# Expert routing tile by tile into lists of token numbers, with blocks gathered by number

## The chip, the cores and the metric

The kernel runs on one core of a Trainium2 chip. It is fp32 throughout: where the matmul wants precision, a number is split into a rounded part ("hi") and a remainder ("lo"), and three products (hi·hi, hi·lo, lo·hi) are added. The metric is the device time of one execution in microseconds (us). The kernel before takes 1038.77 us, the median of 3 runs (1036.66 to 1042.51).

## The reference

Three layers follow each other. Tokens are numbered b·768 + t for 4 batches of 768.

```python
# 1. linear attention with a delta rule, per batch and head (4 x 8 heads of 48), 768 steps
y[t] = q[t] @ state;  v_old = kt @ state;  state += bt * outer(kt, v[t] - v_old)
# 2. dense layer on 3072 tokens of 384
h = x @ w_in; x = np.maximum(0.01 * h, h) @ w_out          # 384 -> 2048 -> 384
# 3. one expert of 8 for each token
logits = x @ w_gate + modality_bias[modality_id]
e_idx = np.argmax(logits, axis=1); gate_w = softmax(logits)[n, e_idx]
for e in range(8):
    mask = e_idx == e
    out[mask] = gate_w[mask, None] * (np.maximum(x[mask] @ w1[e], 0) @ w2[e])   # 384 -> 1024 -> 384
```

The reference's own numbers for these inputs put 3069 tokens on expert 1 and 3 on expert 3; the other six get none. In blocks of 128 tokens that is 24 + 1 = 25 blocks.

## The kernel before

Every engine has an instruction stream written out by hand, with semaphores between them. Two nested loops, `for n, f in slots(): slot(n, f)`, order the first two layers. n is a tile of 512 tokens (6 tiles, `TT`; 128 tokens of each batch), f one of 16 slices of the 2048 hidden features. In slot (n, f) TensorE (PE) runs `up(n, f + 1)` (9 matmuls of 512 columns), pieces of the attention of tile n + 1 and n + 2, and `down(n, f)` (9 matmuls). So attention is spread between the matmuls of the dense layer. The last tile, n = 5, has no attention beside it. After each `up`, ACT scales (`small_h`), DVE takes the maximum (`leaky`), ACT rounds (`round_g`) and DVE makes the remainder (`rest_g`); `down` needs that.

The small steps on PE share three PSUM banks (5, 6, 7) in rotation. `fill(step)` takes the next bank and waits until the step that used it three turns earlier has been drained (`drained0` to `drained2`); the engine that reads the bank signals that. In slot 8 these steps are two W, one Y and two K transposes (KT), in slot 9 two U (`updates`) and two KT.

Routing: `rows_t` and `logits_half` transpose the result of tile n - 1 and compute its logits in slots 0 to 4 of tile n. All other routing waits for the last tile. Then DVE chooses experts for all 24 groups of 128 tokens at once, PE computes ranks, DVE forms each token's row in the sorted order (`pos`), and GpSimd (POOL) writes 24 groups of rows to `sorted_rows` in DRAM, one indirect DMA for each:

```python
for j in range(TOKT):
    pool.indirect_dma_start(out=sorted_rows, out_offset=...(ap=pos[:, j:j + 1], axis=0), in_=row_buf[:, j, :]).then_inc(s.scat, 16)
```

Meanwhile DVE makes the block table (a column per block: expert, count, change, next expert, active, end) and signals `tab_rdy`. SP loads the first expert's weights, waits for all 24 scatters and loads block 0 and block 1.

The expert stage is a loop over blocks of 128 sorted rows. `pe_block(x)` runs `block_up(x)` (18 matmuls), the transposes of the next block `block_t(x + 1)`, `block_down(x - 1)` (24 matmuls) and `block_ht(x)` (8 transposes). DVE and ACT split the results; DVE copies the row's token number and gate to `meta` and signals `meta_rdy`. That lets SP load block x + 2 with one plain DMA, since sorted rows are contiguous. POOL scatters finished rows to `out`. When the expert changes, ACT and DVE split new weights, and POOL takes half of the w2 split.

Of the kernel before, what the change touches and what calls it, by code (L numbers as in the profile page):

```python
# [14 lines left out]
P = 128  # L15
# [26 lines left out]
ROW = DM + 4  # L42
MODS = 2

# [47 lines left out]
def build(nc, q, k, v, beta, moe_w_in, moe_w_out, modality_id, w_gate, modality_bias, w1, w2, out):  # L92
    with ExitStack() as ctx:
# [6 lines left out]
        x2_rows = nc.dram_tensor("x2_rows", [TOKT, P, DM], F32, kind="Internal").ap()  # L100
        wo_lo_d = nc.dram_tensor("wo_lo_d", [FT, P, DM], F32, kind="Internal").ap()
        sorted_rows = nc.dram_tensor("sorted_rows", [(BLOCKS + 2) * P, ROW], F32, kind="Internal").ap()
# [7 lines left out]
        empty_row = sb("empty_row", [P, ROW])  # L110
# [3 lines left out]
        lx = sb("lx", [P, TOKT, EXPERTS])  # L114
        mask = sb("mask", [P, CH])
        after_constants = sb.at
# [11 lines left out]
        x2_t = sb("x2_t", [P, KT, TW])  # L128
        g_hi = [sb(f"g_hi{i}", [P, TW], F32R) for i in range(2)]
        g_raw, g_lo = [], []  # L130
        for i in range(2):
# [25 lines left out]
        mask2 = nc.alloc_sbuf_tensor_at("mask2", [P, P], F32, offset=SB_END - 4 * P)  # L157
        assert sb.at <= SB_END - 4 * P


        sb = Region(nc, attention_at)
        row_buf = sb("row_buf", [P, TOKT, ROW])
        before = sb("before", [P, P])
        ones = sb("ones", [P, P])
        lg, bsel, eq, onehot, within = (sb(x, [P, TOKT, EXPERTS]) for x in ("lg", "bsel", "eq", "onehot", "within"))

        PAD_T, PAD_E = 16, 4
        pref = [sb(f"pref{i}", [P, PAD_T + TOKT, EXPERTS]) for i in range(2)]
        end_sum = [sb(f"end_sum{i}", [P, PAD_E + EXPERTS]) for i in range(2)]
        modf, mod0, mx, total, gate, emin, posf = (sb(x, [P, TOKT]) for x in  # L170
                                                   ("modf", "mod0", "mx", "total", "gate", "emin", "posf"))
        pos = sb("pos", [P, TOKT], I32)
        iota_e = sb("iota_e", [P, EXPERTS])
        iota_i = sb("iota_i", [P, EXPERTS], I32)
        token_id = sb("token_id", [P, TOKT], I32)
        blk_i = sb("blk_i", [P, EXPERTS], I32)
        blk_j = sb("blk_j", [P, EXPERTS], I32)
        blk_n, start, used, last_e = (sb(x, [P, EXPERTS]) for x in ("blk_n", "start", "used", "last_e"))
        NBK = BLOCKS + 1
        bi_i = sb("bi_i", [1, NBK], I32)  # L180
        bi_f = sb("bi_f", [1, NBK])
        be_tmp = sb("be_tmp", [1, NBK, EXPERTS])
        be_tmp2 = sb("be_tmp2", [1, NBK, EXPERTS])
# [1346 lines left out]
```

## Time and profile before

| | |
|---|---|
| median of 3 runs | 1038.77 us |
| profiled execution | 1043.0 us, span 1041.2 us |
| busy share: PE / DVE / ACT / POOL | 87% / 52% / 33% / 6% |
| dense layer ends, first expert matmul | 717.98 us, 773.88 us |
| chain of waits, by engine | PE 73%, DVE 15%, ACT 3% |

All times below are of the profiled execution, from the start of its span. The busy share says who works most over the whole span; which stage a change can shorten is read from the chain of waits and from stretches of time.

### The profile page before, as it was taken

What the parts mean: (1) busy time and instruction counts of PE and PEld (TensorE: products, weight loads), DVE (VectorE), ACT (ScalarE), POOL (GpSimd) and SP (SyncE); (2) the same over time, 40 slices, a digit from 0 to 9 for tenths busy, and PEclk for the clock granted to TensorE, in tenths of its full rate; (3) what the DMA queues carried; (4) which work ended last, traced back from release to release, by engine and by line L of the source; (5) the groups of instructions that cost most, each with busy time, mean ns of one, the idle gap of its engine ahead of it and who ended that gap; (6) DMA issues with size and microseconds to landing.
All of it is one profiled execution on the core that took longest, in us unless ns stands there. A gap on an engine that the chain in (4) does not pass through costs nothing.

```text
span 1041.2 us, 26308 instructions
## 1 busy us (share of the span) xinstructions
PE 910.7 (87%) x10264; PEld 781.9 (75%) x10265; DVE 542.5 (52%) x1455; ACT 344.8 (33%) x608; POOL 66.7 (6%) x79
## 2 busy tenths in 40 slices
PE   5195899989999999999999999998039999999982
PEld 5194678878887888888888887886028999999972
DVE  5947963688249843885378523243523333333341
ACT  4153244433344344424443423333022222222240
POOL 0000000000000000000000000000550101110111
PEclk9677989999999999999999999999559999999995
DMA  9311544454024402351225012250471111111122
GB/s 202 99 35 39 130 126 149 148 151 111 25 55 107 115 26 62 92 123 33 55 63 127 28 32 69 69 197 16 162 265 54 46 38 38 46 38 46 38 91 76
DMA packets 151745, 89.04 MB, mean 86 GB/s; under 512 B 108385, under 2 KB 147809, under 8 KB 151265
## 3 DMA queue, kind: packets, MB, share of 16 engines
q1 hardware_dynamic: 148512, 78.14, 28.0%
q0 software_dynamic: 3136, 9.49, 2.3%
q8 instruction: 75, 1.23, 0.5%
q14 instruction: 22, 0.17, 0.1%
HBM read 59.77 MB, written 23.32 MB: 80 GB/s over the span
## 4 chain that ended last, share of the span: by engine, by line
PE 73%; DVE 15%; ACT 3%; issue 2%; POOL 2%; SPq 1%; DMA 1%; POOLq 0%; DVEq 0%; ACTq 0%
PE bank L462 16%; PE bank L447 15%; PE bank L638 10%; PE bank L614 10%; DVE inv_t L1193 3%; DVE inv_tmp L1187 3%; PE bank L406 2%; PE bank L391 2%; POOL sorted_rows L866 2%; PE bank L624 2%; PE bank L338 2%; PE bank L433 2%; PE bank L430 2%; PE bank L477 2%; PE bank L418 2%
## 5 line engine op out<-in xcount | busy, mean ns | idle before, releaser
L1255 DVE TENSOR_TENSOR g_raw<-bank,g_raw 128x512 f32<-128x512 f32 x96 | 66.2, 689 | 151.7 <-ACT g_raw L963 151.4
L963 ACT ACTIVATE g_raw<-bank 128x512 f32<-128x512 f32 x96 | 57.3, 597 | 250.2 <-PE bank L447 250.2
L462 PE MATMUL bank<-g_hi,wo_hi 128*128 128x512 f32 x288 | 121.9, 423 | 9.5 <-DVE g_lo L1259 7.5
L447 PE MATMUL bank<-x_hi,wi_hi 128*128 128x512 f32 x288 | 117.2, 407 | 12.5 <-DVE x_lo L1251 12.5
L462 PE MATMUL bank<-g_lo,wo_hi 128*128 128x512 f32 x288 | 113.9, 395 | 0.0
L462 PE MATMUL bank<-g_hi,wo_lo 128*128 128x512 f32 x288 | 113.6, 395 | 0.0
L447 PE MATMUL bank<-x_lo,wi_hi 128*128 128x512 f32 x288 | 113.4, 394 | 0.0
L447 PE MATMUL bank<-x_hi,wi_lo 128*128 128x512 f32 x288 | 113.3, 393 | 0.0
L968 ACT ACTIVATE g_hi<-g_raw 128x512 fp32r<-128x512 f32 x96 | 60.6, 631 | 89.7 <-DVE g_raw L1255 89.7
L1259 DVE TENSOR_TENSOR g_lo<-g_raw,g_hi 128x512 fp32r<-128x512 f32 x96 | 66.2, 690 | 41.7 <-ACT g_hi L968 41.6
L638 PE MATMUL bank<-w_hi,ht_hi 128*128 128x384 f32 x200 | 70.4, 352 | 7.6 <-DVE ht_lo L1481 7.2
L1193 DVE TENSOR_TENSOR inv_t<-inv_t,inv_tmp 128x110 f32<-128x110 f32 (+35 forms) x366 | 75.3, 247 | 0.2
L1187 DVE TENSOR_TENSOR inv_tmp<-inv_a,inv_t 128x110 f32<-128x110 f32 (+35 forms) x366 | 74.9, 246 | 0.0
L447 PEld LDWEIGHTS bank<-x_hi,wi_hi 128*128 128x128 f32 x288 | 54.7, 190 | 25.4 <-DVE x_lo L1251 13.4
L462 PEld LDWEIGHTS bank<-g_hi,wo_hi 128*128 128x128 f32 x288 | 54.5, 189 | 23.3 <-issue 9.1
L638 PE MATMUL bank<-w_lo,ht_hi 128*128 128x384 f32 x200 | 68.2, 341 | 0.0
L638 PE MATMUL bank<-w_hi,ht_lo 128*128 128x384 f32 x200 | 68.0, 340 | 0.0
L462 PEld LDWEIGHTS bank<-g_lo,wo_hi 128*128 128x128 f32 x288 | 54.6, 190 | 12.4
L447 PEld LDWEIGHTS bank<-x_hi,wi_lo 128*128 128x128 f32 x288 | 54.7, 190 | 11.9
L614 PE MATMUL bank<-w_hi,xt_hi 128*128 128x512 f32 x150 | 61.7, 412 | 1.6 <-DVE xt_lo L1452 1.2
L447 PEld LDWEIGHTS bank<-x_lo,wi_hi 128*128 128x128 f32 x288 | 54.9, 190 | 10.4
L462 PEld LDWEIGHTS bank<-g_hi,wo_lo 128*128 128x128 f32 x288 | 54.8, 190 | 8.8
(199 smaller groups left out, 1568.5 us busy)
## 6 DMA issues: line engine op xcount, KB each, us to landing
wo_lo<-wo_lo_d SPq DMA_DIRECT2D x80, 192.0 KB, 2.4
w_raw<-in_moe_w SPq DMA_DIRECT2D x6, 1536.0 KB, 7.9
sorted_rows<-empty_row SPq DMA_DIRECT2D x33, 194.0 KB, 2.9
xb<-sorted_rows SPq DMA_DIRECT2D x27, 194.0 KB, 2.4
kq_in_rows<-in_k SPq DMA_DIRECT2D x6, 768.0 KB, 5.2
k_raw<-in_k SPq DMA_DIRECT2D x24, 192.0 KB, 4.1
vals<-in_v SPq DMA_DIRECT2D x24, 192.0 KB, 4.4
kq_in_rows<-in_q SPq DMA_DIRECT2D x6, 768.0 KB, 5.3
```

Source lines behind the costliest of these rows:

```text
L338: mm = pe.matmul(b[half_p(hh), CH * j:CH * j + CH], k_t[head_p(hh), pair, chunk(m // 2)], k_t[head_p(hh), pair, chunk(m // 2)], start=True ...
L391: mm = pe.matmul(b[half_p(hh), HD * j:HD * j + HD], k_t[head_p(hh), pair, chunk(c)], state[c][head_p(hh), pair, :], start=True, stop=True)
L447: mm = pe.matmul(bank[f % 2][:], a[:, m, P * f:P * f + P], x[:, m, :], start=(m == 0 and x is x_hi and a is wi_hi), stop=(m == KT - 1 and ...
L462: mm = pe.matmul(acc[m][:], w[:, P * m:P * m + P], g[f % 2][:], start=(f == 0 and g is g_hi and w is not wo_lo[j % RING]), stop=(f == FT - ...
L614: mm = pe.matmul(bank[2 + h][:], a[par][:, m, :], w[:, m, 512 * h:512 * h + 512], start=(m == 0 and a is xt_hi and w is w1_hi), stop=(m == ...
L638: mm = pe.matmul(bank[6 + par][:, 0:DM], a[:, m, :], w[:, m, :], start=(m == 0 and a is ht_hi and w is w2_hi), stop=(m == KE - 1 and a is ...
L963: act.activation(g_raw[f % 2][:], bank[f % 2][:], ACT.Copy, scale=0.01).then_inc(s.hs_ev, 1)
L968: act.activation(g_hi[f % 2][:], g_raw[f % 2][:], ACT.Copy).then_inc(s.gh_ev, 1)
L1187: made.append(counted(dve.tensor_tensor(tmp[:, a:b, :], inv_a[:, j, j + 1 + a:j + 1 + b].unsqueeze(2).broadcast_to([P, b - a, cols]), inv_ ...
L1193: c = counted(dve.tensor_tensor(rows_t, rows_t, tmp[:, a:b, :], ALU.add))
L1255: dve.tensor_tensor(g_raw[f % 2][:], bank[f % 2][:], g_raw[f % 2][:], ALU.max).then_inc(s.gr_ev, 1)
L1259: dve.tensor_tensor(g_lo[f % 2][:], g_raw[f % 2][:], g_hi[f % 2][:].bitcast(F32), ALU.subtract).then_inc(s.g_rdy, 1)
```

## The change

The choice of expert, ranks and places are done for each tile in the slots of the next tile. Expert e owns a fixed range of a list in DRAM, `id_list`, from e · 4096. `place` turns ranks into list positions with a running `base`, and POOL scatters pairs of token numbers (8 bytes) to these positions, four indirect DMAs a tile. The rows themselves stay in `x2_rows` in DRAM in tile order, now 385 wide with the gate in the last column. A block is read in two steps: SP loads 128 pairs of numbers (`load_ids`), and POOL gathers the 128 rows by number. After five tiles `first_expert` takes the expert with most tokens so far; its weights are loaded and split in the slots of the last tile, and its first two blocks are run without the table. `block_table` follows behind them. POOL's half of the w2 split goes to DVE. The writes of empty rows (33 DMAs) and the reload of `row_buf` are gone.

```diff
+        id_list = nc.dram_tensor("id_list", [LIST, 2], I32, kind="Internal").ap()
@@ tensor
+            def ranks(n):
+                pe.wait_ge(s.picked_rdy, n + 1)
+                b, done = fill(("K", n))
+                pe.matmul(b[:, 0:SUB * EXPERTS], lower[:], picked[:, SUB - 1:, :].rearrange("p a b -> p (a b)"), start=True, stop=False)
+                for d in range(1, SUB):
+                    pe.matmul(b[:, 0:SUB * EXPERTS], ones[:], picked[:, SUB - 1 - d:2 * SUB - 1 - d, :].rearrange("p a b -> p (a b)"),
+                              start=False, stop=(d == SUB - 1))
+                for i in range(SUB):
+                    mm = pe.matmul(b[:, 64:64 + EXPERTS], ones[:], picked[:, SUB - 1 + i, :], start=(i == 0), stop=(i == SUB - 1))
+                mm.then_inc(done, 1)
...
+                late = 0 if n == TT - 1 else 3
+                if n >= 1 and f in (late, late + 1):
+                    logits(n - 1, f - late)
+                if n >= 1 and f == (3 if n == TT - 1 else 8):
+                    ranks(n - 1)
...
+                if n == TT - 1 and f == FT - 2:
+                    pe.wait_ge(s.gr_ev, FT * TT - 1)
+                    block_t(Blk(0, 0))
...
+            logits(TT - 1, 0)
+            logits(TT - 1, 1)
             for i in range(SUB):
                 rows_t(TT - 1, i)
+            ranks(TT - 1)
+            block_up(Blk(0, 0), 1)
+            pe.wait_ge(s.gr_ev, FT * TT)
+            block_t(Blk(0, 1))
...
+            block_ht(0)
+            block_up(Blk(0, 1), 1)
+            block_down(Blk(0, 0), 1)
+            block_ht(1)
+            block_t(Blk(0, 2))
             pe.wait_ge(s.tab_rdy, 1)
+            block_up(Blk(0, 2))
+            block_t(Blk(0, 3))
+            block_down(Blk(0, 1))
+            block_ht(2)
@@ sync
+            def load_ids(x, at):
+                sp.dma_start(ids[x.par][:], id_list[bass.ds(at, P), :]).then_inc(ids_in[x.par], 16)
...
+                if n >= 1 and f == (6 if n == TT - 1 else 11):
+                    store_gates(n - 1)
+                if n == TT - 1 and f == 5:
+                    sp.wait_ge(s.first_rdy, 1)
+                    first = sp.value_load(first_i[0:1, 0:1], min_val=0, max_val=EXPERTS - 1)
+                    load_w1(first)
+                    load_w2(first)
+                if n == TT - 1 and f == 7:
+                    sp.wait_ge(s.scat, 16 * SUB * (TT - 1))
+                    for x in (Blk(0, 0), Blk(0, 1)):
+                        load_ids(x, sp.value_load(first_i[0:1, 1 + x.n:2 + x.n], min_val=0, max_val=LIST - P))
...
-                sp.wait_ge(s.meta_rdy, b + 1)
-                load_block(x.next(2))
+                sp.wait_ge(s.meta_rdy, x.n + 1)
+                load_ids(x.next(2), list_at(sp, x.next(2)))
...
+            load_ids(Blk(0, 2), list_at(sp, Blk(0, 2)))
+            load_next(1, sp.value_load(table[0:1, 3, 0:1], min_val=0, max_val=EXPERTS - 1))
@@ gpsimd
+            def gather(x, rows=TOKENS):
+                pool.wait_ge(ids_in[x.par], x.half * 16 + 16)
+                pool.sem_inc(s.gather_go, 1)
+                pool.indirect_dma_start(out=xb[x.par][:], out_offset=None, in_=x2_rows[0:rows, :], in_offset=bass.IndirectOffsetOnAxis(
+                    ap=ids[x.par][:, 0:1], axis=0), bounds_check=last_token, oob_is_err=False).then_inc(xb_in[x.par], 16)
...
-                        pool_block(Blk(i, d))
+                        gather(Blk(i, d).next(2))
                         scatter(Blk(i, d - 1))
@@ vector
+            def place(n):
...
+                step(dve.tensor_tensor(at_e[:], b[:, 0:SUB * EXPERTS].rearrange("p (a b) -> p a b", b=EXPERTS), over_j(base[:], SUB),
+                                       ALU.add))
+                dve.tensor_tensor(base[:], base[:], b[:, 64:64 + EXPERTS], ALU.add).then_inc(drain(("K", n)), 1)
+                step(dve.tensor_tensor(at_e[:], at_e[:], picked[:, SUB - 1:, :].bitcast(F32), ALU.mult))
+                step(dve.tensor_reduce(posf[:], at_e[:], AX.X, ALU.add))
+                dve.tensor_copy(pos[:, tile], posf[:]).then_inc(s.pos_rdy, 1)
...
+                if n >= 1 and f == (4 if n == TT - 1 else 9):
+                    place(n - 1)
+                if n == TT - 1 and f == 4:
+                    first_expert()
+                if n == TT - 1 and f in (9, 10):
+                    split_w1(f - 9, 1)
+                if n == TT - 1 and f in (11, 12):
+                    split_w2(f - 11, 1)
...
+            relu(0)
+            split_xt(Blk(0, 1))
+            keep_meta(Blk(0, 0))
+            split_ht(0)
+            block_table()
+            relu(1)
+            keep_meta(Blk(0, 1))
+            gated(Blk(0, 0))
+            split_ht(1)
+            split_xt(Blk(0, 2))
```

Three places show how instructions move. The first is PE in slots 8 and 9 of tile 1. Of the kernel before, this is the end of `up(1, 10)`, the two U steps of slot 9, which wait for banks of the rotation (`drained`), and the start of `down(1, 9)`:

```order
L447 MATMUL bank<-x_hi,wi_lo 128x512
L406 MATMUL bank<-vals,inv_s 64x48 [waits drained0,drained2,drained1,td_ev]
L406 MATMUL bank<-vals,inv_s 64x48 x15
L406 MATMUL bank<-vals,inv_s 64x48 [waits drained1,drained0,td_ev]
L406 MATMUL bank<-vals,inv_s 64x48 x15
L462 MATMUL bank<-g_hi_69,wo_hi 128x512 [waits g_rdy,ring1]
```

Of the change, first the end of slot 8's Y step, the ranks (L506 to L511) and the start of `down(1, 8)`, then the same place in slot 9 as above:

```order
L446 MATMUL bank<-qk_t,u_sb 48x64 x2
L506 MATMUL bank<-picked,lower 128x32 [waits drained2,picked_rdy]
L508 MATMUL bank<-picked,ones 128x32 x3
L511 MATMUL bank<-picked,ones 128x8 x4
L475 MATMUL bank<-g_hi_91,wo_hi 128x512 [waits g_rdy,ring0]
```

```order
L460 MATMUL bank<-x_hi,wi_lo 128x512
L419 MATMUL bank<-vals,inv_s 64x48 [waits drained2,drained0,td_ev]
L419 MATMUL bank<-vals,inv_s 64x48 x15
L419 MATMUL bank<-vals,inv_s 64x48 [waits drained0,td_ev]
L419 MATMUL bank<-vals,inv_s 64x48 x15
```

The ranks take one more turn of the rotation, on the bank of `drained2`; two KT steps later the first U step of slot 9 comes to the same bank, and its wait on `drained2` is for the ranks to be drained. In the kernel before, that turn of the bank belonged to the Y step of slot 8, which ACT drains.

The second is DVE in slots 9 and 10 of the same tile. Before, `leaky` (L1255) and `rest_g` (L1259) of slot 9 are followed at once by those of slot 10:

```order
L1255 TENSOR_TENSOR g_raw_71<-bank,g_raw_71 128x512 [waits hs_ev]
L1259 TENSOR_TENSOR g_lo_70<-g_raw_71,g_hi_68 128x512 [waits gh_ev]
L1255 TENSOR_TENSOR g_raw_73<-bank,g_raw_73 128x512 [waits hs_ev]
L1259 TENSOR_TENSOR g_lo_72<-g_raw_73,g_hi_69 128x512 [waits gh_ev]
L1133 COPY diag<-bank 32x256 [waits filled2]
```

Of the change (L1320 is `leaky`, L1324 `rest_g`, L1374 to L1383 `place`):

```order
L1320 TENSOR_TENSOR g_raw_94<-bank,g_raw_94 128x512 [waits hs_ev]
L1324 TENSOR_TENSOR g_lo_93<-g_raw_94,g_hi_91 128x512 [waits gh_ev]
L1374 TENSOR_TENSOR at_e<-bank,base 128x32 [waits picked_rdy,filled2]
L1376 TENSOR_TENSOR base<-base,bank 128x8 [waits route]
L1377 TENSOR_TENSOR at_e<-at_e,picked 128x32
L1378 TENSOR_REDUCE posf<-at_e 128x4 [waits route]
L1379 CAST pos<-posf 128x4 [waits route]
L1381 TENSOR_REDUCE total<-ex 128x4 [waits ex_rdy]
L1382 TENSOR_SCALAR total<-total 128x4 [waits route]
L1383 RECIPROCAL gate<-total 128x4 [waits route]
L1320 TENSOR_TENSOR g_raw_96<-bank,g_raw_96 128x512 [waits hs_ev]
```

The bank of the ranks is drained by L1376, which stands behind `rest_g` of slot 9.

The third is SP in the block loop, between the signal `meta_rdy` and the load that follows it. Before, the row address is known and the block itself is loaded (L788):

```order
L793 UNCONDITIONAL_BRANCH
L802 REGISTER_ALU
L788 ISA [waits meta_rdy]
L788 DMA xb_164<-sorted_rows 128x388
L810 UNCONDITIONAL_BRANCH
```

Of the change:

```order
L840 REGISTER_ALU
L312 ISA [waits meta_rdy]
L312 TENSOR_LOAD table
L312 ISA x2
L757 ISA
L757 DMA ids_140<-id_list 128x2
```

Behind the wait stand a value load and its two checks, and what is loaded is the block's numbers; the block's rows follow by POOL's gather.

## Rows read from the trace of the kernel before

**Rows 1.** The page: busy us (share of the span) and instructions of each engine.
```profile
PE 910.7 (87%) x10264; PEld 781.9 (75%) x10265; DVE 542.5 (52%) x1455; ACT 344.8 (33%) x608; POOL 66.7 (6%) x79
```
**Rows 2.** Stretches: length, busy PE, PEld, DVE, ACT, POOL, granted clock, DMA share, GB/s.
```profile
150.00:640.00 490.00, 484.86 (x6794) 405.04 (x6787) 291.23 (x825) 192.13 (x351) 2.86 (x3) 1.00 0.33 84
718.00:774.00 56.00, 7.74 (x44) 6.85 (x44) 22.73 (x74) 11.13 (x14) 28.62 (x25) 0.59 0.43 151
```
**Rows 3.** Chain of waits, dense layer to experts: start, us, what.
```profile
715.69 2.30 PE bank L462 x9
...
719.73 4.09 PE bank L477 x24
...
769.22 2.49 DMA xb<-sorted_rows
...
773.88 6.87 PE bank L614 x18
```
**Rows 4.** Chain of waits, one block of the expert stage.
```profile
792.22 4.12 PE bank L614 x18
796.33 0.33 PE bank L601 x3
796.66 4.17 PE bank L638 x24
800.83 0.87 PE bank L624 x8
```
**Rows 5.** Slot 9 of tile 1: chain of waits, then DVE's timeline.
```profile
284.06 2.00 PE bank L406 x64
...
286.12 0.69 DVE L1259 TENSOR_TENSOR g_lo<-g_raw,g_hi 128x512 fp32r<-128x512 f32 x1 [0.69 <-ACT g_hi L968]
```
**Rows 6.** Small operations, DVE's timeline: the table runs from 734.58 on.
```profile
723.85 0.19 DVE L1353 COPY lx<-bank 128x32 f32<-128x32 f32 x1 [8.31 <-PE bank L477]
...
734.58 0.17 DVE L1411 TENSOR_SCALAR used<-blk_n 128x8 f32<-128x8 f32 x1
...
744.06 0.17 DVE L1441 CAST table<-at_end 1x32 int32<-1x32 f32 x1
```
**Rows 7.** One block on DVE, SP and POOL, timeline.
```profile
789.08 0.17 DVE L1474 COPY meta<-xb 128x2 f32<-128x2 f32 x1 [0.58 <-issue]
789.45 0.34 SPq L788 DMA_DIRECT2D xb<-sorted_rows  x1
791.38 0.62 DVE L1461 TENSOR_SCALAR o_sb<-bank,meta 128x384 f32<-128x384 f32 x1 [2.13 <-PE bank L638]
...
792.85 1.01 POOL L876 DMA_INDIRECT out<-o_sb,meta  x1 [22.22 <-DVE o_sb L1461]
```
**Rows 8.** DMA issues over the span: count, KB each, us to landing.
```profile
xb<-sorted_rows SPq DMA_DIRECT2D x27, 194.0 KB, 2.4
...
x_rows<-stage SPq DMA_DIRECT2D x20, 192.0 KB, 1.8
...
out<-o_sb,meta POOLq DMA_INDIRECT x25, 2.5
```
**Rows 9.** Line L266, a value load from the table, 770 to 960 us, ns.
```profile
L266 SPq TENSOR_LOAD <-table x19: 263/270/275, 783.5 to 951.7; - x19
```
**Rows 10.** A large load in the last tile, and the ring load behind it.
```profile
row_buf<-x_rows SPq DMA_DIRECT2D x1, 3840.0 KB, 13.0
...
DMA to landing us min/median/max: 9.8/9.8/9.8
```
**Rows 11.** Indirect DMAs beside two weight loads, 740 to 750 us.
```profile
sorted_rows<-row_buf,pos POOLq DMA_INDIRECT x8, 4.9
```
**Rows 12.** Chain of waits: twelve logit matmuls at full clock.
```profile
665.15 1.31 PE bank L477 x12
```
**Rows 13.** DVE's timeline: two halves of w1, later one of w2.
```profile
999.33 3.43 DVE L1488 TENSOR_TENSOR w_lo<-w_raw,w_hi 128x1536 fp32r<-128x1536 f32 x2 [1.78 <-ACT w_hi L1091]
...
1014.20 3.72 DVE L1493 TENSOR_TENSOR w_lo<-w_raw,w_hi 128x1536 fp32r<-128x1536 f32 x1 [2.17 <-ACT w_hi L1079]
```

More of the change, by code:

```diff
@@ new lines, in block_t, with block_up @@
+            def block_t(x):
+                b, par = x.n, x.par
+                pe.wait_ge(xb_in[par], x.half * 16 + 16)
+                if not early(b):
+                    pe.wait_ge(s.xt_rdy, b - 1)
+                for m in range(KT):
+                    mm = pe.transpose(bank[par][:, P * m:P * m + P], xb[par][:, P * m:P * m + P], ident[:])
+                mm.then_inc(s.xt_mm, 1)
+            def block_up(x, count=None):
+                b, par = x.n, x.par
+                count = expert_count(pe, x) if count is None else count
+                pe.wait_ge(s.xt_rdy, b + 1)
+                pe.wait_ge(s.relu_a, b)
+                pe.wait_ge(s.relu_d, b)
+                for h in range(2):
+                    pe.wait_ge(w1l[h], count)
+                    for m in range(KT):
+                        for a, w in ((xt_hi, w1_hi), (xt_hi, w1_lo), (xt_lo, w1_hi)):
+                            mm = pe.matmul(bank[2 + h][:], a[par][:, m, :], w[:, m, 512 * h:512 * h + 512],
+                                           start=(m == 0 and a is xt_hi and w is w1_hi), stop=(m == KT - 1 and a is xt_lo))
+                    mm.then_inc(s.m1_mm, 1)
@@ L489, in slot, with pe_block @@
+            def pe_block(x):
+                block_up(x)
+                block_t(x.next())
+                block_down(x.next(-1))
+                block_ht(x.n)
             def slot(n, f):
@@ L642, in pe_block @@
-            def pe_block(x, first=False):
-                b, par = x.n, x.par
-                block_up(x)
-                block_t(x.next())
-                if not first:
-                    block_down(x.next(-1))
-                block_ht(b)
+            ranks(TT - 1)
+            block_up(Blk(0, 0), 1)
+            pe.wait_ge(s.gr_ev, FT * TT)
+            block_t(Blk(0, 1))
+            for i in range(SUB):
+                pe.wait_ge(*is_drained(("R", TT - 1, i)))
+            pe.wait_ge(*is_drained(("K", TT - 1)))
@@ L1455, in gated @@
+            choose(TT - 1)
+            place(TT - 1)
             def gated(x):
@@ L1460, in gated, with relu @@
                 dve.wait_ge(s.meta_rdy, b + 1)
[L1461 to L1464 removed]
+                dve.tensor_scalar(o_sb[par][:], bank[6 + par][:, 0:DM], meta[par][:, 0:1], None, ALU.mult).then_inc(s.o_rdy, 1)
+            def relu(b):
                 dve.wait_ge(s.m1_mm, b * 2 + 2)
```

728 lines of the change are left out of this document (373 added, 355 removed).

## The prediction

> **What bounds the kernel now.** I read the page first: PE is busy 87% of the span [rows 1]. Which stages the rest lies in comes from the stretches of time. From 150 to 640 us PE is busy 484.86 of 490 us, and from 718 to 774 us only 7.74 of 56 [rows 2]. So the reader should see a program that is limited by PE, with one hole of 56 us. The chain of waits shows what the hole is made of: the dense layer's last matmuls end at 717.98 us (715.69 + 2.30 in the chain, rounded), logits follow, DVE routes all tokens, POOL sends 24 scatters, block 0 is loaded at 769.22, and the first expert matmul starts at 773.88 [rows 3]. After that one block costs 4.12 + 0.33 + 4.17 + 0.87 = 9.49 us, all of it PE [rows 4], 24 times. Work that is put into the first stretch or into the block loop costs what it adds to PE's own chain. Work taken out of the hole pays in full. I sum against the profiled execution's own time of 1043.0 us. It is 4.2 us above the median of the three runs, so at the end I scale by 1038.77/1043.0.
>
> **What the first five tiles pay.** Logits are 24 matmuls a tile as before. New are 8 rank matmuls a tile, of 32 or 8 columns. The trace has no such thing. From above they cost what logit matmuls of 96 columns cost, 1.31/12 = 0.11 us each [rows 12], and from below nothing. I take 0.07, as they are narrower but load the same weights: 0.6 us a tile, 3 us in five tiles (0 to 4.4).
>
> The bank rotation costs more. In tiles 1 to 3 the first U step of slot 9 needs the ranks' bank, and that is drained by the second instruction of `place`, behind `rest_g` of that slot. U started at 284.06, right after `up`; `rest_g` ended at 286.12 + 0.69 = 286.81 [rows 5]. Two small operations behind it (0.19 us for one of 128x32 [rows 6], the second half overlapped) put the drain at 287.1. PE then stands 3.0 us with `down` queued behind U, as it issues in order. Three tiles give 9.1 us. In tile 4 there are no KT steps, so the ranks' bank comes up again only in slot 10, and in tile 5 there is no attention: nothing. The other new work hides. DVE's choice and placing (some 15 operations of 0.2 us a tile [rows 6]) lie in slots 6 and 9, beside PE's attention steps. The scatters of numbers run on an idle POOL. ACT's table changes between exponential and square root come ahead of waits. If that cover were gone, each tile would pay 1 to 3 us. The 33 writes of empty rows freed nothing that PE waited for.
>
> **The last tile.** `place` and `first_expert` are together about 16 dependent steps of 0.2 us [rows 6], 3.3 us. DVE's idle time in a slot and the slack of the `down` chain are together about as long: 0.1 us. SP waits for `first_rdy` before it issues the weights, and the next ring load of `wo_lo` (needed by `down(5, 8)`) is queued behind 3 MB of them. The row to compare is the reload of 3.84 MB in this same tile: it took 13.0 us, and a ring load issued 3.7 us later took 9.8 us, so it landed with it [rows 10]. For 3.07 MB that is 10.7 us from about 679.5, so 690.2, and by my count `down(5, 8)` would start near 689.2: 1 us of stall (0 to 3). Splitting the weights fits into ACT's and DVE's idle time there. So the dense layer ends 3 + 9.1 + 0.1 + 1 = 13.2 us later.
>
> **The hole.** Counted from the end of the dense layer (0). Logits and rows as now until 7.6: copy out 1.75, 24 logit matmuls 4.09 [rows 3], transposes. `choose` (6 steps of 0.2) ends at 7.1, so ranks run at 7.7 and `block_up(0)` starts at 9.0. It is 4.12 us at full clock [rows 4] and ends at 13.1. Relu, split, `keep_meta` and the two halves of `ht_lo` keep DVE until 16.6. Then comes `block_table`, 45 instructions. The present table has 38 in 744.23 - 734.58 = 9.65 us [rows 6], and the new one has more that overlap; I take 10.3 (9 to 11.5), until 26.9. PE meanwhile runs `up(1)` and `down(0)` until 23.2, (13.1, then 0.7 for relu, 0.9 for `block_ht`, 4.1 and 4.2), then waits for relu(1), which stands behind the table on DVE, until 27.6. SP goes on at 27.0: a value load with its checks 0.5 (0.27 is the load [rows 9]), number load 2.2, POOL's start 0.85, gather 4.9, because the next expert's weights are issued right behind (scatters beside such loads took 4.9 [rows 11]). Block 2 is there at 35.5, is transposed and split in 1.5, and `up(2)` starts at 37.0. In the kernel before, `up(2)` starts at 792.22 [rows 4], which is 74.2. That is 37.2 us gained. One part comes back: after a wait of 8 us in the sum the granted clock will be low again, as it was for the present first block, where `up` took 6.87 us [rows 3] and not 4.12: 2.7 us. Net gain 34.5.
>
> **The block loop.** Here a short plain load becomes a chain. Before, `meta` ends at 789.25, the block load is issued at 789.45 and takes 2.4 us, and the transposes need it at 796.33 [rows 4, 7, 8]. So from `meta` to the transposes there are 7.1 us. Now: 0.2 to wake SP, 0.5 for the value load [rows 9], number load 2.2, POOL from signal to issue 0.85 (o_sb ends at 792.00, POOL starts at 792.85 [rows 7]), gather, 0.1 to wake PE. The gather is not in the trace. The indirect scatter to `out` lands in 2.5 us; a plain load takes 0.6 longer than a plain store, 2.4 against 1.8 [rows 8]. So 3.1, with 2.5 and 4.9 as ends. The sum is 6.95 (6.35 to 8.75), and `meta` itself is 0.1 later for one more copy. It just fits, and since `meta(b)` also waits for the transposes of b + 1, each us above 7.1 would be paid by every block. I take 0.05 us a block, 1 us for 21 blocks.
>
> The Trainium skill (DMA: Bandwidth & Descriptors, Anatomy of one DMA, SWDGE path) gives 2.0 us plus bytes/436e3 for a DMA issued by GpSimd, 2.45 us for these 197 KB, and says the wait is longest where the target is HBM. By it the gather would be shorter than the scatter and the loop 0.65 us from its limit. The rows have it the other way for plain transfers, load slower than store, and the sum goes by them.
>
> **The end.** w2 is split by DVE alone: two halves of some 1.7, as w1's, one behind the other, instead of one of 3.72 beside POOL's work [rows 13]. With ACT's halves overlapped `down` starts 1.4 us sooner; but POOL's last gather waits for numbers queued behind a useless weight load and delays the last scatters. Together 0.
>
> **Sum.** 13.2 - 34.5 + 1 = -20.3: 1043.0 becomes 1022.7, and 1018.5 on the scale of the median. I say 1019.
>
> **Rivals.**
> - *The gather does not fit* (chance 0.22). 0.4 to 1.1 us more a block, 8 to 23 us: 1027 to 1042, the middle 1034. For it: there is no margin, and small number loads of 8 bytes a partition are unmeasured. Against: most of my pieces are from quiet rows of the same loop.
> - *The bank wait is shorter or absent* (0.10). Then 6 to 9 us less, 1010 to 1013. For it: U runs one turn after ranks only if the rotation is as I counted. Against: the order shows the same `drained2`.
> - *Slower* (0.08). One mechanism: the gather's landing at the loaded value of 4.9 us in every block. The chain is 8.75 + 0.1, 1.75 us over, times 21 is 37 us: 1055. It decides from about 0.97 us a block, a gather landing of 4.0 us. For it: rows are read in scattered order, beside a scatter. Against: in the quiet loop the scatter's landing is 2.5.
> - The forecast, 1012 to 1026 (0.60).
>
> **How the numbers follow.** About 0.5% is what a measurement of this kernel can tell from no change, 5.2 us. Faster takes the forecast, the bank rival and half and more of the first: 0.60 + 0.10 + 0.13 = 0.83. Same 0.08, slower 0.09. The range goes from 1009, where the bank rival begins, to 1035, the middle of the gather rival: it leaves out about 0.19.
>
> **What would show it.** In the profile after: PE waits of about 3 us at the U step (L419), three times, released by DVE `base`; ranks of 0.5 us or so; the first expert matmul about 9 us after the dense layer; a wait for relu of block 1 of some 4 us and one for the gather of block 2 of some 5; then a block period of 9.5 us. A wait of PE for the DMA of `xb` in each block would mean the gather rival. The prediction would be wrong above all through the landing time of the gather, which counts 21 times, and next through the table's length, which counts once.

## The result, and the profile after

The kernel before takes 1037.80 us (median of 4, 1036.66 to 1042.51), the changed one 1052.86 us (median of 4, 1051.73 to 1055.83). The ratio is 1.0141, 95% interval 1.0101 to 1.0180: slower by 1.4%, where faster by 2% was forecast. The span of the profiled execution goes from 1041.2 to 1052.0 us, 10.8 longer, where the medians are 15.1 apart: the execution profiled before was one of the longer ones of its kernel (1043.0 us against the median of 1037.80), the one profiled after was not (1053.73 against 1052.86). Stretches of the two traces therefore add up to 10.8, and some 4 us of the medians' difference is not in them.

The page of the changed kernel, busy time and granted clock:

```profile
PE 932.5 (89%) x10308; PEld 796.5 (76%) x10309; DVE 551.9 (52%) x1561; ACT 353.1 (34%) x609; POOL 85.8 (8%) x100
...
PEclk9676999999999998999899999998978999999986
```

PE is busy 21.8 us longer than before [rows 1] with 44 instructions more. Longer at nearly the same count points to slower matmuls, so the clock row is the next thing to read, and the waits of PE go with it:

```profile
PE bank L520 <- DMA xb<-x_rows,ids: 9.6, 2, 7.2
PE bank L419 <- DVE base L1376: 9.6, 3, 3.2
...
PE bank L475 <- DMA wo_lo<-wo_lo_d: 6.3, 1, 6.3
PE bank L557 <- DVE ht_lo L1593: 5.8, 1, 5.8
...
PE bank L543 <- issue: 4.0, 1, 4.0
```

The last two are no new losses: both lie in places that the forecast had. The first belongs to the change of expert near the end, where the same wait was 7.2 us before; the second ends at 778.50 us and is the wait behind the block table.

Stretches of the changed kernel, columns as in [rows 2]; the first and the last are whole stages, the three between lie behind a wait of PE:

```profile
150.00:640.00 490.00, 475.82 (x6563) 397.82 (x6555) 294.68 (x878) 196.78 (x345) 18.59 (x19) 0.98 0.34 69
...
289.90:293.30 3.40, 3.40 (x36) 2.92 (x33) 0.00 (x0) 0.95 (x2) 2.65 (x3) 0.50 0.02 1
402.60:409.40 6.80, 6.15 (x70) 5.60 (x71) 1.36 (x9) 0.49 (x1) 4.58 (x5) 0.50 0.01 1
...
716.60:723.40 6.80, 4.32 (x10) 3.45 (x11) 0.00 (x0) 0.00 (x0) 2.05 (x2) 0.50 0.45 130
751.00:790.00 39.00, 24.34 (x128) 20.94 (x128) 17.43 (x73) 8.07 (x16) 5.00 (x5) 0.80 0.31 106
```

Before, the granted clock was 1.00 from 150 to 640 us [rows 2]. Now there are stretches at 0.50, the lower level of 1.2 GHz, of 3.4 us (tile 1) and 6.8 us (tiles 2 and 3), each right behind a wait of 3.2 us, and 6.8 us around the wait for `wo_lo`. Two more, of 3.4 us each, begin at 218.2 us, at the start of tile 1, and at 641.5 us, at the end of tile 4; the kernel before has neither.

I divided both traces at the same events (the start of DVE's `x_lo` of each tile, of the first copy of `x_t` at the end of the dense layer, and of the first matmul of `up` of blocks 2 and 24; before, that of block 2 starts at 791.97 us, 0.25 ahead of its row in the chain [rows 4]). The differences add up to the span's. An ordinary table, in us:

```
                                          before    after   difference  forecast
start to x_lo of tile 1                   215.82   216.26      +0.4        0
tile 1                                    108.91   114.73      +5.8        3.6
tile 2                                    108.88   115.76      +6.9        3.6
tile 3                                    108.90   115.90      +7.0        3.6
tile 4                                    101.97   105.96      +4.0        0.6
tile 5, to the end of the dense layer      73.53    82.64      +9.1        1.7
end of the dense layer to up(2)            73.97    38.42     -35.5      -37.2
up(2) to up(24)                           209.70   215.63      +5.9        3.7
up(24) to the end                          39.52    46.73      +7.2        0
sum                                                           +10.8      -20.3
```

Nearly all of the forecast gain of the hole is there. It was lost again in five other places: slot 9 of tiles 1 to 3, tile 4, the ring load of tile 5, the block loop and the end.

Slot 9 of tile 1, the chain of waits:

```profile
279.46 0.21 PE bank L506
279.67 0.34 PE bank L508 x3
280.01 0.44 PE bank L511 x4
...
283.49 2.07 PE bank L460 x9
285.58 0.61 ACT g_raw L1003
286.21 0.70 DVE g_raw L1320
286.94 0.64 ACT g_hi L1010
287.63 0.57 issue
288.21 0.19 DVE at_e L1374
288.42 0.17 DVE base L1376
288.60 0.14 issue
288.73 2.70 PE bank L419 x64
```

The reader should see: `up` ends at 285.58, U waits until `base` frees the bank and starts at 288.73, and its 64 matmuls then take 2.70 us. At the full clock they took 2.00 [rows 5]. The ranks take 1.0 us (first three rows).

### The profile page after: what moved, and what is told of

It is laid out like the page before. It is cut to its first block, busy times and chain, and to the rows that moved or that the text cites. A ratio compares the mean times of both kernels' runs of the same rounds, so it can differ in the third digit from the quotient of the medians.

```text
span 1052.0 us, 26474 instructions
## 1 busy us (share of the span) xinstructions
PE 932.5 (89%) x10308; PEld 796.5 (76%) x10309; DVE 551.9 (52%) x1561; ACT 353.1 (34%) x609; POOL 85.8 (8%) x100
## 4 chain that ended last, share of the span: by engine, by line
PE 72%; DVE 15%; DMA 4%; ACT 3%; issue 2%; SPq 1%; DVEq 0%; POOLq 0%; POOL 0%; ACTq 0%
PE bank L475 16%; PE bank L460 15%; PE bank L533 9%; PE bank L557 9%; DVE inv_t L1258 3%; DVE inv_tmp L1252 3%; PE bank L419 3%; PE bank L404 2%; PE bank L446 2%; PE bank L443 2%; PE bank L351 2%; PE bank L543 2%; PE bank L497 2%; PE bank L431 2%; DMA wo_lo<-wo_lo_d 1%
## 5 line engine op out<-in xcount | busy, mean ns | idle before, releaser
L1320 DVE TENSOR_TENSOR g_raw<-bank,g_raw 128x512 f32<-128x512 f32 x96 | 66.0, 688 | 161.4 <-ACT g_raw L1003 158.3
L475 PE MATMUL bank<-g_hi,wo_hi 128*128 128x512 f32 x288 | 124.2, 431 | 13.3 <-DMA wo_lo<-wo_lo_d 6.3
L460 PE MATMUL bank<-x_hi,wi_hi 128*128 128x512 f32 x288 | 118.1, 410 | 10.3 <-DVE x_lo L1316 10.3
L1324 DVE TENSOR_TENSOR g_lo<-g_raw,g_hi 128x512 fp32r<-128x512 f32 x96 | 66.2, 689 | 41.7 <-ACT g_hi L1010 40.8
L460 PEld LDWEIGHTS bank<-x_hi,wi_hi 128*128 128x128 f32 x288 | 55.3, 192 | 23.5 <-DVE x_lo L1316 11.4
L882 POOL DMA_INDIRECT id_list<-row_token,pos x24 | 23.7, 986 | 542.9 <-DVE pos L1379 537.4
L460 PEld LDWEIGHTS bank<-x_lo,wi_hi 128*128 128x128 f32 x288 | 55.5, 193 | 10.7
```

Source lines behind the costliest of these rows:

```text
L460: mm = pe.matmul(bank[f % 2][:], a[:, m, P * f:P * f + P], x[:, m, :], start=(m == 0 and x is x_hi and a is wi_hi), stop=(m == KT - 1 and ...
L475: mm = pe.matmul(acc[m][:], w[:, P * m:P * m + P], g[f % 2][:], start=(f == 0 and g is g_hi and w is not wo_lo[j % RING]), stop=(f == FT - ...
L882: pool.indirect_dma_start(out=id_list, out_offset=bass.IndirectOffsetOnAxis(ap=pos[:, j:j + 1], axis=0), in_=row_token[:, j, :], in_offset ...
L1320: dve.tensor_tensor(g_raw[f % 2][:], bank[f % 2][:], g_raw[f % 2][:], ALU.max).then_inc(s.gr_ev, 1)
L1324: dve.tensor_tensor(g_lo[f % 2][:], g_raw[f % 2][:], g_hi[f % 2][:].bitcast(F32), ALU.subtract).then_inc(s.g_rdy, 1)
```

## Experiments

Each is an edit of the changed kernel. Medians are compared with 1052.86 and 1053.62, its two measurements. The runs were spread over four chips: `e1_place8`, `e2_ring`, `e7_fill` and `e8_count` on the first, `e3_tail` to `e6_place_ring` on the second, `e10_best` to `e13_pieces` on the third, `e14_after` to `e17_ranks_twice` on the fourth. The kernel before took 1038.00, 1038.73, 1037.26 and 1038.22 us there. The changed kernel is known to have run on the fourth alone, and the same code (three edits, below) took 1015.95 us there and 1011.11 on the third. So `e10_best` to `e13_pieces` are compared with one another or by segments of their traces, and not by medians with the rest, and for the first two chips too a difference of medians is less sure than a segment of a trace. One segment varies whatever the edit: `x_lo` of tile 1 starts at 214.2 to 216.3 us in most traces, and at 218.6 to 218.8 in those of `e6_place_ring`, `e8_count` and `e16_place_ring`.

### Is it the wait, and does the clock add to it?

**Place one slot earlier.**

```
-                if n >= 1 and f == (4 if n == TT - 1 else 9):
+                if n >= 1 and f == (4 if n == TT - 1 else 8):
                     place(n - 1)
```

> The changed kernel with VectorE's place of tiles 1 to 3 one slot earlier (slot 8, in which the ranks bank is filled, in place of 9). Theory A (each 3.2 us wait of the U matmuls for VectorE's read of that bank costs its length, and a stretch at half the granted clock behind it costs as much again): the 9.6 us of waits go, and so do the half-speed stretches at 289.9 to 293.3, 402.6 to 409.4 and 518.6 to 525.4 (17 us at half speed, 8.5 us lost): 15 to 18 us less, a median of 1035 to 1038. Theory B (only the waits cost; the stretches at half speed are there for another reason and stay): 9.6 less, 1043. Theory C (the tiles are longer because VectorE and ScalarE have more work): the wait moves to another line and the time stays at 1050 or more.

1036.42 us (10 runs), 16.4 less. Tiles 1 to 3 take 111.00, 110.29 and 110.28 us, together 14.8 less. From 150 to 640 us the clock is 1.00, and the waits for `base` are gone. So is the stretch at half clock at the end of tile 4, which takes 103.86 us in place of 105.97 though the edit does not touch it:

```profile
150.00:640.00 490.00, 483.86 (x6727) 404.11 (x6726) 298.23 (x882) 199.91 (x351) 18.59 (x19) 1.00 0.35 69
```

Theory B, 9.6 and no more, is out, and so is C.

**The same wait, filled with work.** Place stays where it was.

```
                     if f == 9:
+                        if n >= 1:
+                            pe.wait_ge(s.gr_ev, FT * n + 10)
+                            for _ in range(14):
+                                pe.matmul(bank[1][:], wi_hi[:, 0, 0:P], x_hi[:, 0, :], start=True, stop=True)
                         updates(n + 1, 1, 0)
```

> The changed kernel with 14 matmuls of 512 columns more in slot 9 of tiles 1 to 3, ahead of the U matmuls, into a bank whose content is no longer needed (extra work with no effect on the output). They fill the 3.2 us in which TensorE stood idle there. If the half-speed stretches behind those waits come from the idle time, they go and the time falls by 5 to 8 us though TensorE has more to do: 1045 to 1048. If they do not, the time stays at 1052 to 1054.

1045.64 us (5 runs), 7.2 less, with 42 matmuls more. Tile 1 as the chain of waits shows it (L595 is the new line), and the stretch where the half clock was:

```profile
284.47 3.17 PE bank L595 x14
287.64 0.02 issue
287.66 2.07 PE bank L419 x64
289.73 2.27 PE bank L475 x9
```

```profile
288.10:291.50 3.40, 3.40 (x64) 3.05 (x61) 0.38 (x3) 0.49 (x1) 2.13 (x2) 1.00 0.01 0
401.00:408.00 7.00, 6.96 (x84) 5.56 (x80) 0.48 (x4) 1.40 (x4) 4.84 (x5) 1.00 0.04 3
```

U starts as late as it did, but PE is busy until then, and the clock stays at 1.00. Tiles 1 to 3 fall by 1.5, 2.0 and 2.2 us: 5.7 us is what the clock alone cost. The Trainium skill (TensorE: Matmul & The Clock Gate, What's actually happening) says that the rate follows how busy the engine has been; the trace agrees (0.50 behind 3.2 us of idle time, 1.00 behind 3.17 us of filler).

**The first weights apart.** w1 in slot 6 behind its ring load, w2 in slot 8, both were in slot 5.

```
-                if n == TT - 1 and f == 5:
+                if n == TT - 1 and f == 6:
                     sp.wait_ge(s.first_rdy, 1)
-                    first = sp.value_load(first_i[0:1, 0:1], min_val=0, max_val=EXPERTS - 1)
-                    load_w1(first)
-                    load_w2(first)
+                    load_w1(sp.value_load(first_i[0:1, 0:1], min_val=0, max_val=EXPERTS - 1))
+                if n == TT - 1 and f == 8:
+                    load_w2(sp.value_load(first_i[0:1, 0:1], min_val=0, max_val=EXPERTS - 1))
```

> The changed kernel with the two weight loads of the fullest expert taken apart in the last tile: w1 behind the ring load of slot 6, w2 behind that of slot 8, in place of both in slot 5. Theory A: the ring load of wo_lo that now takes 14.86 us behind both lands in about half of that, the 6.3 us wait for it and the half-speed stretch behind it (716.6 to 723.4, 3.4 us lost) go, and w2 still lands before its split in slot 11: 9 us less, 1043 to 1045. Rival (1.5 MB ahead is enough to make a ring load late, or the splits of w1 become late, which then delay the g of the slots behind): 0 to 4 us less, with waits for wo_lo in two slots or for w1's load.

1043.07 us (10 runs), 9.8 less. Tile 5 falls from 82.64 to 73.98 us (73.53 before the change). No wait for `wo_lo` is left between 690 and 745 us, and the weights land in 8.6 us (median of the two), in time for their splits. The 8.7 us are the wait of 6.3 and the stretch at half clock around it. The hole is 2.0 us shorter as well (36.43 in place of 38.42): the stretch at half clock that the changed kernel has from 754.1 to 757.5 us is not there, and the 24 logit matmuls of the last tile (`L497`) take 2.92 us, not 4.32.

### Why a block takes longer

**The count read early.** PE reads the register that the down matmuls wait with at the start of a block, in place of behind the transposes, which wait for the gathered rows.

```
             def pe_block(x):
+                count = expert_count(pe, x.next(-1))
                 block_up(x)
                 block_t(x.next())
-                block_down(x.next(-1))
+                block_down(x.next(-1), count)
```

> The changed kernel with the register load that the down matmuls of a block need read at the start of the block, in place of between the transposes and the down matmuls. Theory (a block is 0.19 us longer than before because TensorE's queue stands behind the wait for the gathered rows and reads the register only after it, 0.23 us between transposes and down matmuls): the period of a block goes from 9.68 back to about 9.49, 3 to 4 us less over the loop, 1049. Rival (the down matmuls are slower for another reason, the gather's own traffic): the period stays at 9.68 and the time at 1053.

1047.11 us (5 runs, 1044.73 to 1053.26), 5.7 less; the trace is of the longest of them. In the chain of waits, a block of the changed kernel, and then one with this edit:

```profile
869.60 4.13 PE bank L533 x18
873.73 0.33 PE bank L520 x3
874.05 4.39 PE bank L557 x24
878.45 0.87 PE bank L543 x8
```

```profile
872.09 4.13 PE bank L533 x18
876.22 0.33 PE bank L520 x3
876.54 4.17 PE bank L557 x24
880.71 0.87 PE bank L543 x8
```

Only the third row differs, 4.39 against 4.17, which is what it was before [rows 4]. The starts of `up` of blocks 3 to 23 are 9.54 to 9.85 us apart in the changed kernel, 9.68 in the mean, and 9.50 with this edit up to block 22. From there to block 24 they are 10.06 and 10.79 apart, in place of 9.59 and 10.06: ahead of these `up`, 1.4 us of "issue" stand where 0.3 stood. So the register load costs 0.17 us a block where it stands, and moving it has a price of its own: `up(2)` to `up(24)` falls by 2.1 us, not by 3.4. The end is 1.9 us shorter, for which I have no reason.

**Two orders turned round.** SyncE loads the token numbers ahead of the next weights; VectorE keeps number and gate ahead of the split of w1, and so ahead of the register load and branch that guard it.

```
             def sp_block(x):
                 change = sp.value_load(table[0:1, 2, bass.ds(x.n, 1)], min_val=0, max_val=1)
+                sp.wait_ge(s.meta_rdy, x.n + 1)
+                load_ids(x.next(2), list_at(sp, x.next(2)))
                 with sp.If(change > 0):
                     load_next(...)
-                sp.wait_ge(s.meta_rdy, x.n + 1)
-                load_ids(x.next(2), list_at(sp, x.next(2)))
...
                 split_xt(x.next())
+                keep_meta(x)
                 with dve.If(changes(dve, x.next()) > 0):
                     change_w1(x.next())
-                keep_meta(x)
```

> The changed kernel with two orders of the block loop turned round: SyncE loads the token numbers of the block after next before the next expert's weights, in place of behind them, and VectorE keeps the gate and the number of a block before it splits w1 of the next expert, in place of behind it. Theory A (the tail behind up of block 24 is 7 us longer than before because the last gathers wait for numbers that were late for these two reasons, and GpSimd's scatters stand behind the gathers): the 2.4 us wait of block 25's transposes for its rows and the 6.03 us wait of the last gather go, and 5 to 7 us with them: 1046 to 1048. Theory B (only the wait on TensorE counts, the end is set by TensorE): 2.4 less, 1050 to 1051. Theory C (the tail is longer by the clock at its half level whatever the order): no change, 1052 to 1053.

1042.83 us (10 runs), 10 less, more than any theory had; the block loop and the end alone, in the traces, are 11.4 less. The period is 9.50 from block 3 to block 23, and the time from `up(24)` to the end 38.7 us (39.52 before the change, 46.73 after). Each alone:

> Of the two orders turned round, VectorE's alone: number and gate kept ahead of the split of w1, which also takes the register load and branch from ahead of them. Theory A: in each block the numbers' copy is 0.65 us and the gather 0.3 to 0.5 us earlier, the down matmuls start 4.48 us into the block again, the period is 9.50, 3 to 4 us less over the loop, and the 2.4 us wait of block 25's transposes goes: 1046 to 1048. Theory B (the gain of the two together came from SyncE's order): 1052, period 9.70.

> Of the two orders turned round, SyncE's alone: token numbers ahead of the next weights. It acts on the last blocks alone, where an expert changes. Theory A: it takes away the last gather's 6.03 us wait behind the 3 MB and with it the scatters that stand behind it, but neither the wait of block 25's transposes nor the longer period of a block: 3 to 5 less, 1048 to 1050, period 9.70. Theory B (the end is set by TensorE): no change, 1052 to 1053.

Both ran on the third chip, so segments count. VectorE's order alone (1042.52 us, 4 runs) gives the period back, 9.50, but leaves the end at 46.8; the wait of block 25, which its theory A had going, stays. SyncE's order alone (1047.90 us, 4 runs) leaves the period at 9.50 to 9.95 and shortens the end to 43.6. Only together is it 38.7: block 25's transposes still wait 2.8 us in the first and 2.5 in the second for their rows, and nothing in both. Its rows are late for either of two reasons by itself, so that removing one does not show in this wait. With SyncE's order alone, the numbers of block 25 are issued 2.2 us behind `up(24)`, because `meta` stands behind the split of w1, and the rows land 6.8 us behind it. With VectorE's alone the numbers are issued 3.1 us ahead of `up(24)`, but the gather then runs beside the first useless weight load and takes 7.62 us, and the rows land 7.1 us behind `up(24)`. With both, that load is issued only 8.9 us behind `up(24)`. GpSimd, timeline, first the changed kernel and then the one with both orders:

```profile
1009.93 1.02 POOL L890 DMA_INDIRECT xb<-x_rows,ids  x1 [11.82 <-DMA ids<-id_list]
1011.26 1.03 POOL L926 DMA_INDIRECT out<-o_sb,meta_id  x1 [0.30 <-issue]
1032.70 1.02 POOL L890 DMA_INDIRECT xb<-x_rows,ids  x1 [20.42 <-DMA ids<-id_list]
1034.04 1.03 POOL L926 DMA_INDIRECT out<-o_sb,meta_id  x1 [0.31 <-issue]
1036.57 1.00 POOL L926 DMA_INDIRECT out<-o_sb,meta_id  x1 [1.50 <-issue]
```

```profile
1009.96 1.02 POOL L890 DMA_INDIRECT xb<-x_rows,ids  x1 [5.87 <-DMA ids<-id_list]
1011.29 1.03 POOL L926 DMA_INDIRECT out<-o_sb,meta_id  x1 [0.31 <-issue]
1023.70 1.00 POOL L926 DMA_INDIRECT out<-o_sb,meta_id  x1 [11.38 <-DVE o_sb L1575]
```

The last gather fetches rows that no block uses. In the changed kernel its numbers were issued at 1025.87 behind a weight load at 1024.58 that nothing uses either, and two scatters of results stood behind it in GpSimd's order. SyncE's order takes that away, and by itself it shortens the end by 3.2 us.

### The gather of block 2

**The next weights later.** One wait, `sp.wait_ge(xb_in[0], 32)`, ahead of the first `load_next`.

> The changed kernel with the first load of a next expert's weights (3 MB) held back until the rows of block 2 are gathered. Theory A (the gather of block 2 took 6.51 us in place of 2.1 because it ran beside these loads, and up of block 2 waits for it): the wait of 7.2 us falls to about 3 and up of block 2 starts 4 us earlier: 1048 to 1049. Theory B (the gather is held by something else, the scattered numbers or the rows of the last tile): the wait stays at 7, 1053. The weights themselves are needed 200 us later, so their delay costs nothing by either.

1058.12 us (4 runs), 5 more, so both theories fell. The first half of A held, as the chain of waits shows:

```profile
778.60 3.12 DMA xb<-x_rows,ids
...
786.45 7.26 DMA ids<-id_list
...
794.55 3.17 DMA xb<-x_rows,ids
...
797.77 0.90 PE bank L520 x3
```

The gather of block 2 takes 3.12 us alone, against 6.51, PE's wait falls from 7.2 to 4.1 and `up(2)` starts 34.8 us behind the dense layer, not 38.4. But the numbers of block 3, 1 KB, are now issued behind the 3 MB. They take 7.26 us, and PE waits 8.2 us for the rows of block 3. So PE waits 12.3 us for rows in the two places, and 9.6 in the changed kernel. Issued earlier, the 3 MB had passed while PE waited for block 2 anyway.

### Do they add, and what is left?

> The changed kernel with the edits of two runs that are done, place one slot earlier (16.4 us less by the medians) and the weight loads taken apart (9.8 less). They stand in different tiles, so that their gains should add: 1026 to 1027, against 1038.0 of the kernel before. Rival (a stretch at half the granted clock comes back in another place once TensorE runs without a wait): 1030 to 1034.

1027.25 us (4 runs), as expected.

> All five edits together: place one slot earlier (16.4 less by its run), the first weights taken apart (9.8), the count of the down matmuls read at the block's start (2 to 3 less by the period of a block, 9.70 to 9.59), token numbers ahead of the weights and the gate ahead of the split (2 to 6), the next weights behind the gather of block 2 (4). Sum 34 to 39 less than 1052.9 if they add: 1014 to 1019. If only the first two hold together and the rest lies under other waits: 1026.

1022.32 us (5 runs), 3 to 8 more than expected. The sum counted a gain of 4 for the later weights, which had not been measured then and is a loss: `up(3)` is 6.8 us later behind the dense layer than in `e6_place_ring`, which is without that edit (55.0 against 48.3).

> The three edits that gained by themselves, together: place one slot earlier and the first weights taken apart (1027.25 together), and the two orders of the block loop turned round (1042.83 against 1052.86, 10.0 less). The edit that holds the next weights back (1058.12, 5 more) and the count read at the block's start are left out. If the gains add: 1017 to 1018. If the count's move was worth something beside the earlier gather (period 9.59 with it, 9.53 with the earlier gather alone), this is slower by 1 to 2 us: 1019.

1011.11 us (5 runs), ratio to the kernel before 0.9748 (0.9735 to 0.9762), 6 better than the sum. Whether the edits help one another or the chip differs was tried with four kernels on the fourth chip:

> The changed kernel again, as the measure for the other three of this call, on the same chip as they. If the chips are alike, 1052 to 1053. If the chip of the three edits' run was the faster one, some 5 us less here should it be that chip, and a last attention tile of 102.6 us instead of 105.97.

> Place one slot earlier and the first weights taken apart, against the changed kernel on the same chip. If the gains add as on one chip (16.4 and 9.8): 25 to 27 us less than the changed kernel of this call.

> The three edits, on the same chip. Additive and chips differ: 10 less than the two edits of this call, 35 to 37 less than the changed kernel. Edits help one another: 16 less than the two edits, whatever the chip.

1053.62, 1027.72 and 1015.95 us (4 runs each): 25.9 less, and 11.8 less again. Within 2 us they add, so the rest goes with the chip. Each chip was used on one occasion, so the two can't be told apart. The two traces of the same code are 4.8 us apart, 3.9 of it in tiles 1 to 4. They differ in one place that I can name. From 150 to 640 us, waits of PE on U's line, here in the slower:

```profile
PE bank L419 <- issue: 2.5, 6, 0.5
```

In the faster this row does not exist. "issue" is time in which nothing that the profile shows was waited for. It accounts for half of the difference. What it is stays open, as does the other half. Since the kernel before shows next to no such difference, the changed code seems to be open to something that the old one is not.

> The three edits with the eight ranks matmuls of each tile done twice, the second time over the first (the output is the same). If they cost TensorE their own time (1.0 us a tile where a tile ran at full clock) and nothing else, six tiles make 5 to 6 us more than the three edits. If they are cheap and what remains is clock, 1 us or less more.

1023.39 us (4 runs), 7.4 more, where 5 to 6 were expected. Tiles 1 to 5 grow by 1.0, 1.0, 0.8, 0.9 and 0.8 us. The sixth round stands ahead of the first expert block, where 2.6 us are lost: its own time, and a new stretch of 3.4 us at half clock, some 1.7. So ranks cost their own time, 1.0 us a tile, and they are what is left of tiles 2 and 3 on the faster, third chip: 109.8 against 108.9 before the change.

> The three edits together, and the next expert's 3 MB in four pieces of 768 KB, one behind each of the gathers of blocks 2 to 5, in place of all beside the gather of block 2 (the order of the pieces is written out for these inputs). The gather of block 2 has then the DMA engines to itself (2 to 3 us in place of 6.51) and the numbers of block 3 wait behind one piece (3.5 us) in place of all: up of block 2 starts 4 us earlier and no gather is late: 1013 to 1014, against the same kernel without the pieces. Rival (a piece makes the numbers or the gather of its block late by more than the 1 us that is spare): waits for gathered rows in blocks 3 to 6, 1016 to 1022.

1009.55 us (5 runs), ratio 0.9729 (0.9716 to 0.9742), 1.6 less than `e10_best` on the same chip, where about 4 were expected. The wait of block 2 is 3.8 us in place of 6.7, and one of 0.7 us for gathered rows is new in the blocks behind.

## Why the prediction was wrong, step by step

The gain came as forecast. What failed were prices outside the hole: the half clock behind a wait in slot 9, the ring load behind the weights, the register load in the block loop, and the end. Each of these had been set at nothing or nearly nothing.

**The hole** was right. `up(0)` started 8.7 us after the dense layer (9.0), the table took 9.9 us (10.3), from 767.80 to 777.68, and `up(2)` started 38.4 us after it (37.0). The pieces in between were less exact than their sum: the token numbers landed in 1.69 us, where I had taken 2.2, for which I had no row, and the gather in 6.51, where I had taken 4.9. The first up matmuls were cold, 6.90 us against 4.12, 2.8 lost (2.7).

**The bank rotation**, "three tiles give 9.1 us", was right as a wait, 9.6. What failed is the price of a wait: I charged a cold clock in the hole and nowhere else. `e7_fill` shows 5.7 us of it in these tiles. Together 15.3, and `e1_place8` gave 14.8 back in these tiles.

**Ranks**, 0.6 us a tile, measure 1.0. I took them cheaper than logits matmuls because of their few columns; eight of them take 0.99 us (0.21 + 0.34 + 0.44), which is 0.12 each. Five tiles make 5.0 us, a little over the upper end of my range (4.4).

**Tile 4**, +4.0 where 0.6 was forecast, is ranks (1.0), some 1.1 us of "issue" in the last Y matmuls around 639 us, and a stretch at half clock from 641.5 to 644.9 right behind. `e11_ids` and `e12_meta` touch nothing there and have 102.6 on the third chip, the faster one, `e3_tail` and `e4_w_later` have 104.3 on theirs. Why the "issue" time and this stretch come and go is open.

**The ring load**, "1 us of stall (0 to 3)", cost 6.3, and 2.4 of clock behind it. The changed kernel between 703 and 719 us, from the view of its DMAs and as a stretch, and then the reload's stretch in the kernel before:

```profile
DMA packets 2643, 3.67 MB, mean 229 GB/s; under 512 B 900, under 2 KB 2259, under 8 KB 2643
...
w_raw<-in_moe_w SPq DMA_DIRECT2D x2, 1536.0 KB, 13.2
```

```profile
703.00:719.00 16.00, 9.75 (x42) 7.45 (x41) 4.84 (x7) 4.12 (x7) 1.69 (x2) 0.92 0.90 229
```

```profile
679.00:692.00 13.00, 13.00 (x59) 10.74 (x58) 5.38 (x11) 3.69 (x6) 0.00 (x0) 1.00 1.02 355
```

SP issued the weights at 703.1, which is within a us of the forecast when both are counted from `x_lo`, and PE came to need `wo_lo` when I said. The row that I took for the rate was the wrong one; scaled rightly it gives 10.4 us for the two loads of 1536 KB, not 10.7, so the miss is a little larger. With the reload 355 GB/s moved, with the weights and the small packets beside them (900 of 2643 under 512 bytes, among them the gates') 229. Whether the small packets are the reason was not tried. The ring load was issued at 704.18 and landed 14.86 us later.

**The block loop**, "it just fits, 0.05 us a block": the gather did fit. PE waits for no rows in blocks 3 to 24. The number load was shorter than taken, too (1.7, not 2.2), and the gather landed in 3.1 us (3.0 to 3.2), as taken from the rows, and not in 2.45. The rows landed 3.4 to 3.7 us into a block, 0.5 to 0.8 ahead of the transposes at 4.2. But the period rose by 0.17 us, 3.4 us in all, because my chain ended at the transposes. The register load of the down matmuls stands behind the same wait in PE's queue, so rows that come too shortly before they are needed delay what stands behind them. `e8_count` (that load moved) and `e12_meta` (the numbers' copy 5.9 us into a block and not 6.6, the rows 3.0 to 3.3) each bring 9.50 back.

**The end**, "together 0", was +7.2. I had seen the gather behind the useless load, and that it delays the last scatters, and set that off against a gain of 1.4 us without a price. That gather costs 3.2 us (`e11_ids`, end at 43.6). The other 4.9 come back only with both orders (`e3_tail`, 38.7): most of them are the rows of block 25, 2.4 us late, and the half clock behind that wait (the next 24 down matmuls take 5.98 us, and 4.18 in `e3_tail`). My sum had no term for that.

Of the rivals, none was this. The slower one (gather at 4.9 us in every block) did not happen; the time came out slower by several prices at once. Summed with the measured prices, 33.2 - 35.5 + 5.9 + 7.2, the same steps give the +10.8 of the traces.

## What to carry to other kernels

Moving work out of a hole into an engine's full stretch is paid there at the price of its worst effect, not of its busy time: a wait of 3 us in a fully busy TensorE stage also costs 1.5 to 2.2 us of clock behind it, each time, so look first for the slot in which the bank that is waited for can be freed earlier. In a queue that works in order, ask for each small urgent transfer what large one is issued ahead of it: 1 KB of numbers took 1.7 us alone and 7.3 behind 3 MB. When each of two causes alone makes the same transfer late, removing one leaves its wait as it was; try both together before you acquit either.

## What the runs showed of the hardware that I had not expected

- Clock: idle times of 3.2 us were followed by 3.4 or 6.8 us at 1.2 GHz. With the same 3.2 us filled by 14 matmuls it stayed at 2.4 GHz.
- Eight matmuls of 8 or 32 columns with weights of 128x128 take 0.99 us, 0.12 each, no less than one of 96 columns, 0.11 [rows 12].
- A gather of 128 rows from DRAM by number lands in 3.1 us alone and 6.5 beside 3 MB of loads (7.6 beside the one weight load of `e12_meta`).
- Two stretches in which 4.61 and 3.67 MB were moved, mostly large loads, had 355 and 229 GB/s.
- The same code differs by 0.5% between two chips, used on one occasion each (1015.95 and 1011.11 us), on which the kernel before differs by 0.1%.
